# Four pairs of 64-row matmuls in place of eight full-array ones, in a convolution and two top-1 mixture-of-experts layers

## What is computed

```python
logits = x @ w_gate
expert_idx = np.argmax(logits, axis=1)
...
for e in range(E):
    mask = expert_idx == e
    h = np.maximum(x[mask] @ w1[e], 0.0)          # 192 -> 1024
    out[mask] = gate_w[mask, None] * (h @ w2[e])  # 1024 -> 192
```

## Time and profile before

| | us |
|---|---|
| median of 3 runs | 1430.34 |
| lowest, highest | 1422.12, 1433.67 |
| the profiled execution | 1426.65 |
| its span, first to last instruction | 1425.1 |
| layer 0, first to last hidden matmul's stretch | about 275 to 860 |
| layer 1 | about 890 to 1425 |

### The profile page before, as it was taken

One profiled execution on the slowest core, in us unless ns is written; L12 is line 12 of the kernel. 1 busy time (PEld: TensorE's weight loads), 2 busy tenths in 40 slices (PEclk: granted clock), 3 DMA queues, 4 the chain that ended last, 5 costly groups with the idle time before them and its releaser, 6 DMA issues.

```text
span 1425.1 us, 38152 instructions
## 1 busy us (share of the span) xinstructions
PE 1248.3 (88%) x13162; PEld 1169.3 (82%) x13162; DVE 860.8 (60%) x2298; ACT 641.3 (45%) x1126; POOL 445.0 (31%) x476
## 2 busy tenths in 40 slices
PE   2876763299989999999999991999999999999998
PEld 2765663298979998999999990899999999999997
DVE  3787885358978998887777774333333333333332
ACT  3666664045545555554444441333333333333332
POOL 1366777412323333322222222122222222222222
PEclk9666655599999999999999995999999999999999
DMA  8388674928585858561515113462425525125510
GB/s 232 103 254 265 199 224 145 261 65 218 149 235 141 251 146 240 144 203 42 146 40 148 40 35 94 115 156 44 137 63 142 128 64 152 44 44 151 152 44 16
DMA packets 204695, 194.94 MB, mean 137 GB/s; under 512 B 147359, under 2 KB 179771, under 8 KB 199522
## 3 DMA queue, kind: packets, MB, share of 16 engines
q1 hardware_dynamic: 176352, 127.72, 34.8%
q0 software_dynamic: 26096, 64.50, 14.5%
q10 hardware_dynamic: 2194, 2.06, 0.5%
HBM read 101.38 MB, written 70.80 MB: 121 GB/s over the span
## 4 chain that ended last, share of the span: by engine, by line
PE 72%; DVE 12%; DMA 6%; issue 4%; another core or an unknown queue 2%; ACT 2%; POOL 2%; SPq 1%; POOLq 0%; DVEq 0%; ACTq 0%
PE bank L720 70%; DMA wslot<-image 3%; DVE am L943 2%; PE bank L725 2%; POOL rows L466 2%; DVE split L1027 1%; DVE wslot L1054 1%; DVE wam L1012 1%; DVE split L1030 1%; DMA image<-split 1%; DMA stage<-in_moe_w 1%; DVE rowab L952 1%; ACT conv L564 0%; ACT rowt L564 0%
## 5 line engine op out<-in xcount | busy, mean ns | idle before, releaser
L720 PE MATMUL bank<-xT,wslot 128*128 128x256 f16 x5040 | 639.5, 275 | 59.2 <-DMA xT<-rows 50.1
L1114 DVE SCALAR_TENSOR_TENSOR hl<-bank,hh 128x512 f16<-128x512 f32 x504 | 347.7, 690 | 417.6 <-ACT hh L653 372.6
L720 PEld LDWEIGHTS bank<-xT,wslot 128*128 128x128 f16 x5040 | 485.5, 99 | 110.0 <-DMA xT<-rows 50.2
L653 ACT ACTIVATE hh<-bank 128x512 f16<-128x512 f32 x504 | 300.6, 596 | 535.9 <-PE bank L720 529.6
L720 PE MATMUL bank<-wslot,hh 128*128 128x192 f16 x4032 | 541.0, 246 | 0.4 <-DVE hl L1114 0.4
L720 PE MATMUL bank<-wslot,hl 128*128 128x192 f16 x2016 | 496.7, 246 | 0.0
L720 PEld LDWEIGHTS bank<-wslot,hh 128*128 128x128 f16 x4032 | 369.8, 98 | 11.8 <-issue 0.8
L552 POOL DMA_INDIRECT out_tokens<-y,idxt x126 | 122.5, 972 | 416.6 <-ACT y L664 348.6
L487 POOL DMA_INDIRECT rows<-rowt,idxp x126 | 130.1, 1032 | 358.0 <-PE bank L720 197.7
L720 PEld LDWEIGHTS bank<-wslot,hl 128*128 128x128 f16 x2016 | 197.6, 98 | 0.1
L466 POOL DMA_INDIRECT rows<-rowab,idxa x96 | 109.3, 1138 | 61.7 <-issue 46.1
(11 more groups left out here) (137 smaller groups left out, 873.9 us busy)
## 6 DMA issues: line engine op xcount, KB each, us to landing
wslot<-image SPq DMA_DIRECT2D x32, 1024.0 KB
wslot<-image SPq DMA_DIRECT2D x32, 768.0 KB
image<-split POOLq DMA_DIRECT2D x18, 512.0 KB
image<-split SPq DMA_DIRECT2D x8, 1024.0 KB
image<-split POOLq DMA_DIRECT2D x9, 768.0 KB
xw<-in_x SPq DMA_DIRECT2D x4, 1536.0 KB
stage<-in_moe_w SPq DMA_DIRECT2D x8, 768.0 KB
image<-split SPq DMA_DIRECT2D x8, 768.0 KB
```

What stands on the lines that cost most here:

```text
L653: nc.scalar.activation(hh[:, c, :], bank[c][:, :], ACT.Relu).then_inc(hh_out, 1)
L720: return nc.tensor.matmul(o, a, b_, start=start, stop=stop, skip_group_check=True)
L1114: V.scalar_tensor_tensor(hl[:, c, :], bank[c][:, :], 0.0, hh[:, c, :], ALU.max, ALU.subtract).then_inc(hl_out, 1)
```

## The change

`xT` gets a fourth chunk, loaded by a transpose of its own from the f16 columns 64 to 191 of the rows: on partitions 64 to 127 it holds the high parts 128..191, which chunk 1 has on 0 to 63. (Its partitions 0 to 63 are not used.) `x_loaded` now counts 32 a tile.

The product of section 3 leaves `hidden`, which keeps four matmuls for each u, and goes into `hidden_low`, called at the head of the tile for chunks 0 and 1, and ahead of hidden 2 for chunks 2 and 3. For each u it issues one matmul on partitions 0 to 63 (x chunk 1) into `bank[c]` and one on 64 to 127 (x chunk 3) into `bank[c + 1]`. It starts the banks' accumulation. Before it, it waits for `hl_out` of chunk c + 1 of the tile before. The product of the low part of w1 with the low part of x, for elements 128..191, which the full-array matmul had included, is no longer computed.

```diff
-        xT = sb("xT", [P, XS, 3, T], f16)
+        xT = sb("xT", [P, XS, 4, T], f16)
...
-                    sp.dma_start_transpose(xT[:, s, :, :], tile_rows.bitcast(f16)[:, 0:3 * P]).then_inc(x_loaded[s], 16)
+                    sp.dma_start_transpose(xT[:, s, 0:3, :], tile_rows.bitcast(f16)[:, 0:3 * P]).then_inc(x_loaded[s], 16)
+                    sp.dma_start_transpose(xT[:, s, 3:4, :], tile_rows.bitcast(f16)[:, DB:DB + P]).then_inc(x_loaded[s], 16)
...
-                def hidden(t, k, s, x, i, c):
+                def hidden_low(t, k, s, x, i, c):
 
                     if c == 0:
-                        pe.wait_ge(x_loaded[x], (i + 1 + l * NX[x]) * 16)
+                        pe.wait_ge(x_loaded[x], (i + 1 + l * NX[x]) * 32)
                         pe.wait_ge(w_loaded[0][s], (k + 1 + l * NS[s]) * 16)
+                    if late(t, 1):
+                        pe.wait_ge(hl_out, (l * NT + t - 1) * NP + c + 2)
+                    for u in range(2):
+                        for half, xc in ((0, 1), (1, 3)):
+                            part = slice(half * DB, (half + 1) * DB)
+                            f0 = 3 * F + (2 * (c + half) + u) * P
+                            mm(bank[c + half][:, u * T:(u + 1) * T], wslot[part, s, f0:f0 + P],
+                               xT[part, x, xc, :], u == 0, False)
+
+                def hidden(t, s, x, c):
+
                     for u in range(2):
                         f0 = (2 * c + u) * P
                         wcol = lambda w: wslot[:, s, w * F + f0:w * F + f0 + P]
                         o = bank[c][:, u * T:(u + 1) * T]
-                        for n, (w, xc) in enumerate(((0, 0), (0, 2), (1, 1), (2, 0), (3, 1))):
-                            last = mm(o, wcol(w), xT[:, x, xc, :], n == 0, n == 4)
+                        for n, (w, xc) in enumerate(((0, 0), (0, 2), (1, 1), (2, 0))):
+                            last = mm(o, wcol(w), xT[:, x, xc, :], False, n == 3)
                     last.then_inc(h_done, 1)
...
-                    hidden(t, k, s, x, i, 0)
+                    hidden_low(t, k, s, x, i, 0)
+                    hidden(t, s, x, 0)
...
-                        hidden(t, k, s, x, i, c)
+                        if c == 2:
+                            hidden_low(t, k, s, x, i, 2)
+                        hidden(t, s, x, c)
```

## The result

| | before | changed |
|---|---|---|
| median of 20 runs each, us | 1432.76 | 1444.96 |
| lowest, highest | 1422.0, 1445.92 | 1436.54, 1459.93 |
| profiled execution, span | 1425.1 | 1438.2 |

The ratio is 1.0094, 95% interval 1.007 to 1.0118: 13 us slower, where 17 us faster was forecast. Ratios leave out runs that took over 1.5% longer than the fastest of the same kernel, so they can differ a little from the quotient of the medians. (The kernel before has a median of 1417 to 1433 us in the different sets of runs, so a ratio is always against its runs in the same set.)

The account below looks back on a forecast made before the run. TensorE's matmul stream was taken to bound both expert layers. Blocks -20.7 us plus transposes +4.0 made -16.7 us, from a median of 1430.34 to 1413 us; range over all 1377 to 1468, the forecast's own 1401 to 1431.

Parts of the forecast that it names:

- rival 2: At each switch between full array and halves, earlier matmuls must finish: 1469 us, or 1518 with weights loaded after; chance 0.24.
- rival 3: In the blocks the halves run one after the other: 1434 us, or 1462 with switches of 55 ns; chance 0.12.
- rival 4: VectorE or SP takes over in layer 0: hl waits or late xT give back 15 us, 1428 us; chance 0.05.
- The stream bounds both layers, only its pitch counts: TensorE in both expert layers: an unbroken matmul stream, paid by pitch, 109 ns per 256-column and 82 per 192-column matmul.
- Halves run together, a pair in one slot: In a block, two 64-row matmuls share one slot: 218 ns for two pairs, plus 26 ns lag once a block.
- A switch costs 55 ns: Changing between full array and halves, two changes a block, 55 ns each: block 354 ns against 436, 20.7 us gained.
- The low bound from the earlier trace: Switch price of 0: where the matmul kind changes in that trace, the pitch runs on without a gap.
- the upper bound: Switch price of 262 ns: the next full matmul waits 164 ns for the last record's end, then 98 for its weights.
- The new transpose, 4 us: One more DMA a tile on SP: free inside a layer, about 2 us at each layer's start, 4 us in both.
- The new waits cost nothing: Earlier waits for hl at the blocks cost nothing: slack 1.85 us for chunk 1, 3.2 us for chunk 3.
- Late next: more cover for the row transposes, weights for 0.2 us: Layer 0: row transposes' cover goes from 3.06 to 3.19 us; three weight waits swallow under 0.2 us of TensorE's gain.
- rival 1: Switching between full array and halves is free: 54.9 us gained, less 4, giving 1379 us; chance 0.26.

## Why the prediction was wrong

The range held the time (1444.96 in 1377 to 1468) and the direction was wrong. It held it by luck: its upper part was there for rivals 2 and 3, and of the cause of most of the loss the rivals had only a trace, in rival 4. Between the forecast of -17 us and the measured +13 lie 30 us; 19 are the price of the blocks, the rest is mostly the stall in layer 0.

- *The stream bounds both layers, only its pitch counts:* right for layer 1 and for layer 0 from about 610 us. For layer 0's first half it was too simple: the earlier trace rows showed small waits, and I took them for small slack costs instead of asking how near the chain behind them was to stalling. The waits for `rowt` were already 3.8 us in five places, the longest 2.4; I looked at one of 0.28 us.
- *Halves run together, a pair in one slot:* right. The halves start 3 ns apart, where I took 26 once a block; the pair takes 119 ns in place of 109. The Trainium skill ("TensorE: Matmul & The Clock Gate", Part 3) gives about 4 ns for the first, and the trace agrees.
- *A switch costs 55 ns:* the mis-sized term. It measured 96 at the entry and 93 at the exit, 105 by the run with twice the switches. A block costs 430 ns, not 354, so 252 x 6 = 1.5 us are won and not 20.7, and a tile of layer 1 takes 8.31 us and not 8.17. The low bound from the earlier trace rows was no witness: none of those changes splits the array. My value rested on columns passing the array; the weight loads that don't run ahead across a switch stood only in the upper bound. The Trainium skill's sentence ("TensorEngine Tiling (Array Packing)", Tiling Modes) that changing the mode drains TensorE agrees with what is seen; the price is the trace's.
- *The new transpose, 4 us:* right in size. Its issue takes 1.14 to 1.17 us at the layers' starts (1.15 in the middle of all, 4.16 at most). From the first x issue of a layer to the head of tile 1 it is 13.25 us (12.03 before) in layer 0 and 14.33 (12.53) in layer 1, 3.0 us in all; the run with the transpose alone lost 4.
- *The new waits cost nothing:* right, 0.9999 (0.9969 to 1.0028).
- *Late next: more cover for the row transposes, weights for 0.2 us:* wrong, and this is the other step that failed. I counted the cover between an eviction and TensorE's use of its rows, and not what the moved evictions do to the queues of the others: VectorE's placing 0.2 us later, GpSimd's staging load behind it, and a DMA that then takes some 4 us longer. The order alone costs 12 to 14 us, and moving the staging load takes 9 of the 13 away.
- *Rivals:* 1 and 3 are out. Rival 2 had the right kind of price for a switch, and its decision point of 88 ns lies just under the measured 95, but it alone gives +2.5 us with the transposes. Rival 4 named VectorE taking over in layer 0 with 15 us; it was given 0.05, and it named the wrong trigger (hl, xT).

By the terms: -1.5 (blocks) + 3 to 4 (transposes) + 9 to 14 (stall) makes 10.5 to 16.5 us; 13 was measured. The parts, each measured to some 4 us, don't add up more closely than that.

What stays open: why the packets of x come ahead of the staged weights when the staging DMA starts 0.2 us later, why that slows it so much, and why in the changed kernel they did not in one of the three places.

## What to carry to other kernels

Count the switches between the full array and its halves, at some 95 ns each here, against what each block of pairs saves (2 x 109 - 119 = 99 ns a pair): two pairs between two switches were an even trade, four pairs won 0.2 us a tile. Before moving work inside a tile, follow each eviction that moves through the engines' queues to the DMAs that they trigger, and look at whether large transfers then start in another order or distance; an engine-bound stream with a few microseconds of waits can have a chain beside it that is a few tenths from stalling. When a change has parts, time the order alone with the old instructions: here it separated a break-even edit from a stall of 12 to 14 us.

## What was not expected of the hardware

- No weight load runs ahead across a change between full-array and half-array matmuls: the first load after it starts with its matmul (idle 0.16 and 0.21 us on the load row), in all 125 blocks looked at, and each change costs 93 to 105 ns.
- A transpose of one chunk of 256x128 holds SP for 1.15 us, about as long as one of three chunks (1.24 us; both medians, the latter's from 0.70 up): the issue time does not follow the size here.
- A 768 KB staging DMA took 11.5 to 15.5 us in eight of nine cases when it was issued 1.16 to 1.19 us behind a 1 MB weight load, and at most 10.1 when issued 0.94 to 1.03 us behind it. In the eight, 224 to 608 of the x transpose's 256-byte packets went ahead of it, else at most 22.
